# Two half-height streams: every TensorE matmul of a two-network kernel split over the upper and the lower 64 rows

## What is computed

```
# 1. mixing: every token is a weighted sum of itself and the six before it, per head (8 heads of 24)
w = softmax(weight_gen, over the 7 taps);  out[b,s,h,:] = sum_k w[b,s,h,k] * x_pad[b,s+k,h,:]
# 2. gated network, 192 -> 1536 -> 192
xn = x / sqrt(mean(x*x) + 1e-6) * rms_g
g = xn @ w_gate;  x = (g * sigmoid(g) * (xn @ w_val)) @ w_out
# 3. second network, 192 -> 2048 -> 192
h = x @ w_in;  return (h * sigmoid(1.702 * h)) @ w_out2
```

## Time and profile before

| | |
|---|---|
| Time, median of 3 runs | 1330.92 us (1329.9 to 1331.2) |
| Span of the profiled execution | 1328.2 us; the program's time is given for the runs only, and the median lies 2.7 us above this span |
| PE / PEld busy | 1283.0 us (97%) / 1088.3 us (82%) |
| DVE / ACT / POOL busy | 782.2 / 679.0 / 101.7 us |
| A block in the steady state | 79.76 us |

### The profile page before, as it was taken

The page is one execution under the profiler, slowest core; times in us unless marked ns, Lnnn a source line. Parts: engine busy times, 40 slices in busy tenths (PEclk is TensorE's granted clock), DMA queues, the critical chain, the costliest instruction groups (busy, mean ns, idle before and its releaser), DMA issues.

```text
span 1328.2 us, 19585 instructions
## 1 busy us (share of the span) xinstructions
PE 1283.0 (97%) x6304; PEld 1088.3 (82%) x6304; DVE 782.2 (59%) x1186; ACT 679.0 (51%) x1194; POOL 101.7 (8%) x104
## 2 busy tenths in 40 slices
PE   0889999999999999999999999999999999999998
PEld 0667888889888888888889888888888889888898
DVE  5889475473846638475473846638475473843432
ACT  2343646555464553646555454553645555464454
POOL 6873000000000000000000000000000000000000
PEclk9999999999999999999999999999999999999999
DMA  5331000000100001000000100001000000000000
GB/s 141 87 108 39 1 16 31 16 31 4 41 0 15 30 3 41 0 15 30 15 30 3 41 0 15 30 3 41 0 15 30 15 30 0 12 0 13 1 13 13
DMA packets 14525, 32.21 MB, mean 24 GB/s; under 512 B 1828, under 2 KB 7842, under 8 KB 14496
## 3 DMA queue, kind: packets, MB, share of 16 engines
q1 hardware_dynamic: 14496, 31.85, 7.6%
HBM read 25.55 MB, written 6.29 MB: 24 GB/s over the span
## 4 chain that ended last, share of the span: by engine, by line
PE 92%; DVE 1%; issue 1%; ACT 0%; DVEq 0%
PE acc L754 15%; PE up_ps L706 11%; PE up_ps L713 11%; PE up_ps L714 11%; PE up_ps L707 11%; PE up_ps L710 11%; PE acc L755 7%; PE acc L734 3%; PE acc L731 3%; PE acc L735 3%; PE acc L732 3%; PE acc L733 3%; PE acc L768 0%; DVE hidden L654 0%; PE acc L772 0%
## 5 line engine op out<-in xcount | busy, mean ns | idle before, releaser
L669 DVE TENSOR_TENSOR h_lo<-hidden,h_hi 128x512 fp32r<-128x512 f32 x448 | 315.7, 706 | 382.0 <-ACT h_hi L487 381.5
L487 ACT CAST h_hi<-hidden 128x512 fp32r<-128x512 f32 x448 | 278.7, 622 | 186.1 <-DVE hidden L654 178.5
L754 PE MATMUL acc<-out_w,h_hi 128*128 128x384 f32 x1024 | 306.4, 355 | 0.0
L755 PE MATMUL acc<-out_w,h_lo 128*128 128x192 f32 x1024 | 257.6, 252 | 0.0
L471 ACT ACTIVATE hidden<-up_ps 128x512 f32<-128x512 f32 x256 | 153.2, 598 | 203.2 <-PE up_ps L714 202.9
L466 ACT ACTIVATE silu<-up_ps 128x512 f32<-128x512 f32 x192 | 114.5, 596 | 196.1 <-PE up_ps L714 195.7
L654 DVE TENSOR_TENSOR hidden<-silu,up_ps 128x512 f32<-128x512 f32 x192 | 131.8, 687 | 129.0 <-ACT silu L466 128.8
L755 PEld LDWEIGHTS acc<-out_w,h_lo 128*128 128x128 f32 x1024 | 195.0, 190 | 10.2
L754 PEld LDWEIGHTS acc<-out_w,h_hi 128*128 128x128 f32 x1024 | 192.2, 188 | 10.6
L706 PE MATMUL up_ps<-x_hi,up_w 128*128 128x512 f32 x384 | 154.5, 402 | 3.1 <-DVE hidden L654 2.0
L713 PE MATMUL up_ps<-x_rest,up_w 128*128 128x512 f32 x384 | 152.7, 398 | 3.8 <-DVE x_rest L593 3.8
(11 more groups left out here) (80 smaller groups left out, 1671.1 us busy)
## 6 DMA issues: line engine op xcount, KB each, us to landing
x_win<-in_x_dram SPq DMA_DIRECT2D x14, 960.0 KB
out_dram<-out_sb SPq DMA_DIRECT2D x15, 384.0 KB, 2.3
stage<-in_moe_w_out_dram SPq DMA_DIRECT2D x13, 192.0 KB, 2.5
logits<-in_weight_gen_dram SPq DMA_DIRECT2D x16, 112.0 KB, 2.0
stage<-in_moe_w_in_dram SPq DMA_DIRECT2D x4, 256.0 KB, 2.9
stage<-in_moe_w_in_dram SPq DMA_DIRECT2D x8, 128.0 KB, 2.9
stage<-in_moe_w_val_dram SPq DMA_DIRECT2D x3, 256.0 KB, 4.2
stage<-in_moe_w_val_dram SPq DMA_DIRECT2D x6, 128.0 KB, 2.8
```

The lines of the kernel that those rows point to most:

```text
L487: nc.scalar.copy(h_hi[:, u % 4, :], hidden[:, u % 2, :]).then_inc(hi_ready, 1)
L669: nc.vector.tensor_tensor(h_lo[:, u % 4, :], hidden[:, u % 2, :], h_hi[:, u % 4, :].bitcast(F32), ALU.subtract).then_inc(lo_ready, 1)
L754: nc.tensor.matmul(acc[:, j, 0:2 * D], h_hi[:, n % 4, tile], w, start=n == 0, stop=False)
L755: ins = nc.tensor.matmul(acc[:, j, 0:D], h_lo[:, n % 4, tile], w[:, 0:D], start=False, stop=n == U2 - 1)
```

## The change

Each matmul over 128 rows becomes two over 64 rows: `top` takes weights and data of rows 0 to 63, `low` those of rows 64 to 127, both add into the same bank, but never at the same time. TensorE's program is a sequence of slots, each a top and a low matmul that belong to different banks: the low half of a bank runs six slots after its top half, and waits for it on a semaphore (`top_up`, `top_down`, `top_tile`).

The up tiles go in pairs (gate and value of a unit, or two units of the second network). The low parts of the rest weights of both tiles share one array, `pair_lo`: rows 0 to 63 for the pair's second tile, 64 to 127 for its first; `x_twin` and `y_twin` hold the high parts of the rest inputs in rows 64 to 127 for it. A pair takes nine top and nine low matmuls.

The first output begins with the rest bank and then takes the main one; the second output handles two units at once, on two banks at a time (top on one, low on the other, then swapped). The transposes are halved too. Units, waits and the places of the emptyings move: y is emptied at U1 + 3, x still split at U1 + 2. The hardware loops are written out.

```diff
-    EVAC_O, SQUARE, SPLIT_Y, X_T, EVAC_Y, SPLIT_X = 1, 8, 8, U1 - 1, U1 + 1, U1 + 2
+    EVAC_O, EVAC_Y0, SQUARE, SPLIT_Y, X_T, SPLIT_X, EVAC_Y, LAST_Y = 1, 2, 8, 8, U1 - 1, U1 + 2, U1 + 3, U1 + 4
+    TOP, LOW = slice(0, P // 2), slice(P // 2, P)
+    TOP_TILES, LOW_TILES = (2, 0, 3, 1), (3, 1, 2, 0)
...
-        up_w = sb("up_w", [P, 2 * U1 + U2, 4, P], F32R)
+        up_w = sb("up_w", [P, 2 * U1 + U2, 3, P], F32R)
+        pair_lo = sb("pair_lo", [P, PAIRS, P], F32R)
...
# DVE, split_rest
                 nc.vector.tensor_copy(rest[0:REST, :], f32[0:REST, 1, :]).then_inc(hi_sem, 1)
+                nc.vector.tensor_copy(twin[REST:P, :], f32[0:REST, 1, :])
...
# DVE, run: at the head of a unit, ahead of its h_lo
+                    if i > 1 and i < GROUPS and u == EVAC_O:
+                        empty_o(i - 2)
+                    if i == GROUPS and u == LAST_Y - 1:
+                        empty_o(i - 2)
+                    if 0 < i < GROUPS and u == EVAC_Y:
+                        empty_y_rest(i)
...
                     if mixing and u == (U1 - 1 if i == 0 else SPLIT_X):
                         split_x(i + 1)
+                    if i == GROUPS - 1 and u == LAST_Y:
+                        split_last_y(i)
...
# TensorE
+            def top(ps, w, data, start=False, stop=False):
+                return nc.tensor.matmul(ps, w[TOP], data[TOP], start=start, stop=stop)
+            def low(ps, w, data, start=False, stop=False):
+                return nc.tensor.matmul(ps, w[LOW], data[LOW], start=start, stop=stop)
...
+            def low_pair(i, p, k):
+                if k == 0:
+                    pe.wait_ge(top_up, 2 * pair_at(i, p) + 1)
+                    low(a[:, :], wa[:, 0, :], hi)
+                elif k == 1:
+                    low(a[:, :], wa[:, 1, :], hi)
+                elif k == 2:
+                    low(a[:, :], wa[:, 0, :], lo)
+                elif k == 3:
+                    low(a[:, :], wa[:, 2, :], rest)
+                elif k == 4:
+                    low(a[:, :], pair_lo[:, p, :], twin, stop=True).then_inc(
+                        gate_done if p < U1 else up_done, 1)
...
+            def low_tail(before, k):
+                i, p, down = before
+                if down is None:
+                    low_pair(i, p, 3 + k)
+                elif k == 0:
+                    low_pair(i, p, 8)
+                else:
+                    low_down1(*down, k - 1)
+            def step(i, p, before, down=None):
+                for k in range(6):
+                    top_pair(i, p, k)
+                    if before is not None:
+                        low_tail(before, k)
+                for k in range(3):
+                    top_pair(i, p, 6 + k)
+                    low_pair(i, p, k)
+                if down is not None:
+                    for k in range(5):
+                        top_down1(*down, k)
+                        low_pair(i, p, 3 + k)
+                return i, p, down
+            def down2(i, p):
+                pe.wait_ge(lo_ready, unit_at(i, U1 + 2 * p + 1) + 1)
+                visits, ends = 4 * down2_at(i, p), p == U2 // 2 - 1
+                for v in range(4):
+                    at_top, at_low = TOP_TILES[v], LOW_TILES[v]
+                    if v >= 2:
+                        pe.wait_ge(low_tile, visits + v - 1)
+                        pe.wait_ge(top_tile, visits + v - 1)
+                    elif p:
+                        pe.wait_ge(low_tile, visits - 1 + v)
+                        pe.wait_ge(top_tile, visits - 1 + v)
+                    elif i < GROUPS and v == 0:
+                        pe.wait_ge(x_scaled, min(i * 2 + 4, 2 * GROUPS))
+                        if i > 1:
+                            pe.wait_ge(out_ready, i * 2 - 2)
+                    elif i < GROUPS:
+                        pe.wait_ge(main_out, i + 1)
+                        pe.wait_ge(rest_out, i + 1)
+                    else:
+                        pe.wait_ge(out_ready, i * 2 - 3 + v)
+                    for n in (2 * p, 2 * p + 1):
...
+                        top(acc[:, at_top, 0:2 * D], h[:, t], w, start=first)
+                        low(acc[:, at_low, 0:2 * D], h[:, q], w, start=first)
+                        t_last = top(acc[:, at_top, 0:D], h_rest[:, t], w[:, 0:D], stop=last)
+                        q_last = low(acc[:, at_low, 0:D], h_rest[:, q], w[:, 0:D], stop=last)
...
# TensorE's order, block i: down1 of u - 2 in step u; turn_x; then
+                for p in range(U2 // 2 if i else 0):
+                    if p < 2 and i < GROUPS:
+                        before = step(i, U1 + p, before, (i, U1 - 2 + p))
+                    elif p < 2:
+                        before = step(i, U1 + p, before)
+                        down2(i - 1, U2 // 2 - 2 + p)
+                    else:
+                        before = step(i, U1 + p, before)
+                        down2(i, p - 2)
```

More of the change, by code:

```diff
@@ L121, in staged_count, with even_splits @@
         return sum(32 if chunks[q][1] == "rest" else 16 for q in range(c + 1) if place_of(q) == place_of(c))
+    def even_splits(n):
+        return sum(chunks[q][0] is w_in and chunks[q][1] == "rest" for q in range(n + 1))
     def chunks_for_up(m, gated):
@@ L170, in mix_and_two_ffns @@
         y_hi, y_lo, y_rest = (sb(n, [P, N], F32R) for n in ("y_hi", "y_lo", "y_rest"))
+        x_twin, y_twin = sb("x_twin", [P, N], F32R), sb("y_twin", [P, N], F32R)
         silu = sb("silu", [P, 2, N])
@@ L233, in tap_product, with all_blocks @@
                     p.broadcast_to([P, end - first, HEADS, HEAD]))
-        def pairs(ap):
-            return ap.rearrange("p (a b c) -> p a b c", a=2, b=2)
-        def all_blocks(engine, run):
+        def all_blocks(run):
             run(0, range(U1), True)
-            run(1, range(UNITS), True)
-            run(2, range(UNITS), True)
-            with engine.Fori(3, GROUPS - 1) as i:
+            for i in range(1, GROUPS - 1):
                 run(i, range(UNITS), True)
@@ L319, in _ @@
             load_x(3)
-            with sp.Fori(2, GROUPS - 2) as i:
+            for i in range(2, GROUPS - 2):
                 load_logits(i + 2)
@@ L389, in _ @@
                 split_chunk(n, True)
-            with pool.Fori(2, GROUPS) as g:
+            pool.wait_ge(chunk_split, len(chunks))
+            for g in range(2, GROUPS):
                 rms(g)
@@ L436, in scale_x, with empty_main @@
                 ins.then_inc(x_scaled, 1)
[L438 to L446, removed]
+            def empty_main(g):
+                if g:
+                    act.wait_ge(y_ready, g * 2)
+                act.wait_ge(low_down, 2 * down1_at(g, U1 - 1) + 2)
+                nc.scalar.copy(y_f32[:, 0, :], acc_main).then_inc(main_out, 1)
@@ L472, in run @@
                                              ACT.Gelu_apprx_sigmoid).then_inc(gelu_done, 1)
[L473 to L478, removed]
+                    if 0 < i < GROUPS and u == EVAC_Y:
+                        empty_main(i)
                     if u < U1:
@@ L655, in run @@
                                                 ALU.mult).then_inc(prod_done, 1)
[L656 to L661, removed]
                     steps = MIX_SLOT.get(u, []) if mixing else []
-                    if u != EVAC_O and steps:
+                    if steps:
                         mix_step(i + 1, steps[0])
@@ L738, in down2 @@
-            def down2(i, n, tiles=range(STEP)):
-                if is_block(i, 1):
-                    pe.wait_ge(chunk_split, chunks_for_down(n, False))
-                pe.wait_ge(lo_ready, unit_at(i, U1 + n) + 1)
-                if n == 0 and is_block(i, GROUPS):
-                    pe.wait_ge(out_ready, i * 2 - 2)
-                elif n == 0:
-                    pe.wait_ge(main_out, i + 1)
-                    pe.wait_ge(rest_out, i + 1)
-                    pe.wait_ge(x_scaled, 2 * GROUPS if is_block(i, GROUPS - 1) else i * 2 + 4)
-                w = out_w2[:, n, :, :].rearrange("p v d -> p (v d)")
-                for j in tiles:
-                    tile = slice(j * P, (j + 1) * P)
-                    nc.tensor.matmul(acc[:, j, 0:2 * D], h_hi[:, n % 4, tile], w, start=n == 0, stop=False)
-                    ins = nc.tensor.matmul(acc[:, j, 0:D], h_lo[:, n % 4, tile], w[:, 0:D], start=False,
-                                           stop=n == U2 - 1)
-                ins.then_inc(down_done, 1)
+            def top(ps, w, data, start=False, stop=False):
+                return nc.tensor.matmul(ps, w[TOP], data[TOP], start=start, stop=stop)
@@ new lines, in low_down1 @@
+            def low_down1(i, m, k):
+                w, h, h_rest = out_w1[:, m, :, :], h_hi[:, m % 4, :], h_lo[:, m % 4, :]
+                before, last = 2 * down1_at(i, m), m == U1 - 1
+                if k == 0:
+                    pe.wait_ge(top_down, before + 1)
+                    low(acc_rest, w[:, 2, :], h)
+                elif k == 1:
```

(36 more changed lines are left out.)

425 lines of the change are left out of this document (256 added, 169 removed).

## The result

The changed kernel takes 1348.66 us (1347.85 to 1349.73, 4 runs) against 1330.94 (medians): 1.0139 times as long by the estimate over the runs, interval 1.0124 to 1.0154; the two medians by themselves give 1.0133. Forecast were 1312 us and a gain. The sign is wrong, and the time lies outside the forecast's own 1290 to 1328. It lies inside the full range of 1238 to 1448, but only because that range reaches to slower rivals (loads in turn, each half paying its own 21 ns) that did not happen: that is luck. The slots and the steady wait came out as forecast; what was left out is the half clock behind TensorE's standstills, and the new order's cost in the head, that is before the transposes for group 2.

A forecast was written before the change was run, and what follows sets the result against it. TensorE's matmul starts were taken as the bound. Terms -75.0 + 2.8 + 4.8 + 47.6 + 0.9 = -18.9 us took the span from 1328.2 to 1309.3; with 2.7 outside it, 1312 us (own range 1290 to 1328, full 1238 to 1448).

The forecast's parts named there:

- loads in turn: Rival, second output: weight loads of the halves go one after the other; 1384 to 1464 us, centre 1425, chance 0.25.
- each half paying its own 21 ns: Rival, all slots: the 21 ns beyond streaming are paid per half, +81 us; 1382 us, up to 1430, chance 0.10.
- The slots: Up projections: a top and a low half together cost one full matmul, 0.2344 us; 320 fewer, -75.0 us.
- the steady wait: Second output, blocks 1 to 14: TensorE waits 3.4 us for y, emptied behind the split of x; +47.6 us.
- The block without waits: Steady block if TensorE never waits for y: 75.4 us; as a rival 1264 us, chance 0.16 shared with faster slots.
- no overlap: Rival, all matmuls: top and low halves do not run side by side; about 2440 us, chance 0.06.
- The twelve half transposes: Start of each block: six transposes become twelve half ones, 0.3 us more per block, +4.8 us.
- the clock falls in the wait: Rival, after each standstill for y: seven matmuls at half clock, +19 us; 1331 us, chance 0.07.
- The head: First 130 us: POOL's added waits taken as hidden, and no cost entered for the new order there.
- The end: Last blocks: block 15 waits 0.1 us, block 16 about +0.9 us, and six low halves run without a partner.

The follow-up runs named there:

- y_early: The changed kernel with y emptied at unit 14 instead of 15 (EVAC_Y = U1 + 2), ahead of the split of x: 1275.32 us, ratio 0.9585.
- y_early_ten_slots: y_early with the tenth visit put back, one top and one low half-height matmul issued twice per up pair: 1342.14 us, ratio 1.0090.
- y_early_head: y_early with block 0's last two output units right behind group 1's transposes, and y of group 0 out at unit 0 of block 1: 1268.82 us.

## Why the prediction was wrong

*The slots: right, to a few tenths.* The block without waits was forecast at 75.4 us and is 75.33 in y_early. That they agree within 0.1 is in part luck, as two small errors cancel. Loads of a top and a low half start together, like the matmuls; the rivals "loads go one after the other", "each half pays its own 21 ns" and "no overlap" are out. The twelve half transposes take 0.34 us (543.86 to 544.20), less than the 0.57 for six, where 0.3 more was taken: the block has 0.5 us less from them, and as much more elsewhere. Part of this stands at the changes of banks in the second output, where the step to the next group is 0.36 and not 0.29 (y_early, 525.26 to 525.62).

*The wait for y: right,* 3.4 forecast, 3.50 measured, in its place and by its cause; taking it away, and putting it into the kernel before, shows it.

*The step that failed is that the rival "the clock falls in the wait" was left out of the sum.* It was put outside the sum, with a chance of 0.07, and priced at seven matmuls a time, 7 x 0.19 = 1.3 us. A steady block is forecast at 75.38 + 3.4 = 78.8 us; it took 80.65, so 1.87 us more, 24.3 us over 13 blocks, and the rows above place that at half clock behind the standstill. The price was too low as well: blocks with 3.4 us at half clock pay 80.26 - 75.33 - 3.50 = 1.4 us, those with 6.8 us pay 2.4 to 2.9. The argument against it, that the stretch before 40.00 was idle for far longer, said nothing of 3.5 us. (The granted clock could not have told of that stretch: it reads 1.00 there, while the starts 0.42 us apart are the 1.2 GHz level.) With y_early both go: 80.65 - 75.33 = 5.3 us a block, 3.5 wait and 1.8 clock. The wait by itself would have left a gain: 4.4 us saved a block, 3.5 lost. The clock's 1.8 turns the sign, already without the head (1309.3 + 24.3 = 1333.6 us, against a span of 1328.2 before).

*The head is the second miss: its new order was costed at nothing.* Up to the transposes for group 2, 128.0 us follow from the forecast's terms (130.5 less 13 slots, plus transposes) and 138.96 were measured, 10.9 more. y_early_ten_slots, with as many matmul visits as before, also takes 141.32 us there against 130.47, so most of it comes with the new order and not with the number of visits. TensorE waits 4.8 us for x there, because the ten output slots that had filled this stretch moved behind it; then 4.5 us for y of group 0, which those slots finish; and the clock is down for part of the time (0.88). y_early_head, which moves the slots back, takes 5.9 us of it away. The split of what is left between x, mixing and the weights' split was not tested.

*The end*, behind the transposes for group 15, took 160.2 us against 157.2 by the forecast's terms. y_early, without block 14's wait and fall, takes 154.7 us for it, 5.5 less; the wait is 3.5 of that, so the clock is 2.0 of the 3.0 us. The other 1.0 stays open.

In sum: 1309.3 + 24.3 + 10.9 + 3.0 = 1347.5, against a span of 1347.6 us. The three terms are what was measured over the forecast, so the sum shows only that no stretch is left out.

## What to carry to other kernels

When a change moves the order of an engine that is far from busy (DVE 59%), lay the turn from one stage to the next out on all engines: here two instructions behind a 2.5 us split were worth 5.3 us a block, more than the change's whole gain, and one constant turned 1.4% slower into 4.1% faster. Where a TensorE that is otherwise always busy stands still for 2 us or more, allow for the half clock behind it as well: here 1.6 us more behind most waits of 2.13 us, 1.4 to 2.9 behind all of 3.50 (1.8 in the mean), nothing behind 1.06. And follow the work that used to fill a wait: moved elsewhere, it leaves the wait open.

## What the hardware showed that was not expected

Two half-height fp32r streams ran side by side at the full rate, loads included: 0.23 to 0.24 us for two halves of 512 columns, as for one full matmul. In the steady blocks the clock fell behind all standstills of 3.5 us, behind none of 1.06 us, and behind nine of 13 of 2.13 us in one and the same kernel, so the same wait has two prices there. The length of a single wait does not settle it: in the head of y_early_head the clock fell behind two waits, of 0.7 and 1.7 us. What decides between the cases no run here shows.
